# Attention values: three of six key tiles multiplied in one full precision matmul instead of two rounded ones

## The reference

```python
    mask = q_bucket[:, :, :, None] == k_bucket[:, :, None, :]
    scores = scale * np.matmul(q, k.transpose(0, 1, 3, 2))
    scores = np.where(mask, scores, -1000000000.0)
    scores = scores - np.max(scores, axis=-1, keepdims=True)
    attn = np.exp(scores)
    attn = attn / (np.sum(attn, axis=-1, keepdims=True) + 1e-09)
    return np.matmul(attn, v).astype(np.float32)
```

## Time and profile before

| what | value |
|---|---|
| three runs | 1694.59, 1698.58, 1700.28 us |
| their median | 1698.58 us |
| profiled execution, first to last instruction (span) | 1694.0 us |
| lowest of the three runs less that span | 0.6 us |
| mean granted TensorE clock | 0.980 of full |
| attention stage | about 20 to 298 us of the span |

### The profile page before, as it was taken

How to read it: one execution, slowest core, us unless ns; L and a number is a source line. 1 busy time by engine, 2 the same in 40 slices (tenths; PEclk the granted TensorE clock), 3 DMA queues, 4 the chain that set the end, 5 groups by cost and what they waited for, 6 DMA issues and landing times.

```text
span 1694.0 us, 21627 instructions
## 1 busy us (share of the span) xinstructions
PE 1591.6 (94%) x7588; PEld 1310.1 (77%) x7589; DVE 670.9 (40%) x1227; ACT 505.0 (30%) x943; POOL 309.6 (18%) x381
## 2 busy tenths in 40 slices
PE   7999998789999999999999999999999992699997
PEld 6888887568888888888888888888888871577775
DVE  6999998541211211211221121121122134554324
ACT  5887877301111111111111111111111133643213
POOL 3333341320030030030030030030030004322202
PEclk9999999999999999999999999999999995899999
DMA  5343343110110110020020020010011013753310
GB/s 136 92 119 93 104 124 123 51 50 1 50 50 1 50 50 0 15 84 0 0 99 0 0 99 0 0 65 34 0 50 50 1 50 131 271 176 133 134 43 23
DMA packets 49380, 108.06 MB, mean 64 GB/s; under 512 B 7350, under 2 KB 13494, under 8 KB 49344
## 3 DMA queue, kind: packets, MB, share of 16 engines
q1 hardware_dynamic: 44208, 96.30, 17.3%
q10 hardware_dynamic: 2736, 4.98, 1.0%
q0 software_dynamic: 2400, 6.31, 1.0%
HBM read 81.58 MB, written 13.40 MB: 56 GB/s over the span
## 4 chain that ended last, share of the span: by engine, by line
PE 80%; DVE 7%; issue 5%; ACT 3%; DMA 3%; POOL 2%; DVEq 0%; ACTq 0%; POOLq 0%; SPq 0%
PE psum L353 24%; PE psum L355 23%; PE psum L354 23%; PE psum L576 2%; DVE pt_lo L1069 2%; DMA w_raw<-in_moe_w_dram 2%; DVE row_max L1079 1%; PE psum L528 1%; ACT prob L846 1%; PE psum L784 1%; PE psum L565 1%; ACT pt_hi L839 1%; PE psum L566 1%; PE psum L589 1%; PE psum L590 1%
## 5 line engine op out<-in xcount | busy, mean ns | idle before, releaser
L936 ACT ACTIVATE h_hi<-psum 128x512 fp32r<-128x512 f32 x192 | 114.9, 599 | 871.8 <-PE psum L355 871.8
L353 PE MATMUL psum<-xt_lo,w_hi 128*128 128x512 f32 x768 | 304.8, 397 | 0.0
L355 PE MATMUL psum<-xt_hi,w_lo 128*128 128x512 f32 x768 | 301.6, 393 | 0.0
L353 PE MATMUL psum<-w_lo,h_hi 128*128 128x512 f32 x768 | 299.5, 390 | 1.6 <-issue 1.6
L354 PE MATMUL psum<-xt_hi,w_hi 128*128 128x512 f32 x768 | 299.4, 390 | 0.0
L355 PE MATMUL psum<-w_hi,h_lo 128*128 128x512 f32 x768 | 299.1, 390 | 0.0
L354 PE MATMUL psum<-w_hi,h_hi 128*128 128x512 f32 x768 | 298.8, 389 | 0.0
L1232 DVE SCALAR_TENSOR_TENSOR h_lo<-psum,h_hi 128x512 fp32r<-128x512 f32 x192 | 132.7, 691 | 347.9 <-ACT h_hi L936 347.5
L1262 DVE SCALAR_TENSOR_TENSOR tok<-psum,route,tok 128x512 f32<-128x512 f32 x96 | 65.7, 745 | 436.4 <-PE psum L355 436.4
L379 POOL CAST w_hi<-w_raw 128x512 fp32r<-128x512 f32 x64 | 39.2, 612 | 813.4 <-PE psum L355 813.4
L355 PEld LDWEIGHTS psum<-xt_hi,w_lo 128*128 128x128 f32 x768 | 144.6, 188 | 33.8
(11 more groups left out here) (227 smaller groups left out, 2020.5 us busy)
## 6 DMA issues: line engine op xcount, KB each, us to landing
w_raw<-in_moe_w_dram SPq DMA_DIRECT2D x32, 2048.0 KB, 8.0
k_hh<-k_t SPq DMA_DIRECT2D x32, 192.0 KB, 4.0
x_sorted<-zeros SPq DMA_DIRECT2D x21, 257.0 KB, 4.6
x_row<-x_sorted ACTq DMA_DIRECT2D x19, 256.0 KB
k_raw<-in_k_dram SPq DMA_DIRECT2D x16, 192.0 KB, 2.4
q_raw<-in_q_dram SPq DMA_DIRECT2D x16, 192.0 KB, 2.5
v_raw<-in_v_dram SPq DMA_DIRECT2D x16, 192.0 KB, 3.7
k_b<-k_t SPq DMA_DIRECT2D x16, 192.0 KB, 4.3
```

The source lines that it names most:

```text
L353: pe.matmul(acc, a[0], b[1], start=start, stop=False)
L355: return pe.matmul(acc, a[1], b[0], start=False, stop=stop)
L936: act.activation(h_s[0][:, f, :], psum[:, f % 4, :], ACT.Relu).then_inc(m1.h_hi, 1)
```

## The change

The rounded and rest parts `pt_hi` and `pt_lo` are kept only for key tiles 0 to 2. Key tiles 3 to 5 are copied by ScalarE without rounding into a new float32 tile `pt_b`, VectorE's residue for them falls away, and their two rounded matmuls become one plain float32 matmul per key tile. The bank of key tiles 3 to 5 is released by ScalarE's copy instead of VectorE's residue.

```diff
-    pt_hi = [place(f"pt_hi{u}", [P, IT, HALF], F32R, at) for u in range(2)]
-    pt_lo = [place(f"pt_lo{u}", [P, IT, HALF], F32R, at) for u in range(2)]
+    pt_hi = [place(f"pt_hi{u}", [P, IT // 2, HALF], F32R, at) for u in range(2)]
+    pt_b = [place(f"pt_b{u}", [P, IT // 2, HALF], F32, at) for u in range(2)]
+    pt_lo = [place(f"pt_lo{u}", [P, IT // 2, HALF], F32R, at) for u in range(2)]
...
                 if not at_first(g):
-                    pe.wait_ge((s_lo_a, s_lo_b)[c], g)
+                    pe.wait_ge((s_lo_a, s_hi_b)[c], g)
...
             if part == 0:
-                pe.wait_ge(s_lo_b, 3 * hn + 3)
+                pe.wait_ge(s_lo_a, 3 * hn + 3)
+                pe.wait_ge(s_hi_b, 3 * hn + 3)
                 pe.wait_ge(s_v_split, n + 1)
                 pe.wait_ge(s_o_t, hn + 1)
             for j in (2 * part, 2 * part + 1):
+                if j >= IT // 2:
+                    mm = pe.matmul(psum[:, 6, 0:HALF], v_s[u][:, j, :].bitcast(F32), pt_b[half][:, j - IT // 2, :],
+                                   start=False, stop=(j == IT - 1))
+                    continue
                 pe.matmul(psum[:, 6, 0:HALF], v_s[u][:, j, :], pt_lo[half][:, j, :], start=(j == 0), stop=False)
-                mm = pe.matmul(psum[:, 6, 0:HALF], v_s[u][:, j, :], pt_hi[half][:, j, :], start=False,
-                               stop=(j == IT - 1))
+                mm = pe.matmul(psum[:, 6, 0:HALF], v_s[u][:, j, :], pt_hi[half][:, j, :], start=False, stop=False)
...
-                act.copy(pt_hi[half][:, 3 * c:3 * c + 3, a:a + P],
+                act.copy((pt_hi, pt_b)[c][half][:, :, a:a + P],
                          psum[:, 4 + c, 0:HALF].rearrange("p (j i) -> p j i", j=3)).then_inc((s_hi_a, s_hi_b)[c], 1)
...
-            for c in range(2):
-                dve.wait_ge((s_hi_a, s_hi_b)[c], g + 1)
-                dve.tensor_tensor(pt_lo[half][:, 3 * c:3 * c + 3, a:a + P],
-                                  psum[:, 4 + c, 0:HALF].rearrange("p (j i) -> p j i", j=3),
-                                  pt_hi[half][:, 3 * c:3 * c + 3, a:a + P].bitcast(F32),
-                                  ALU.subtract).then_inc((s_lo_a, s_lo_b)[c], 1)
+            dve.wait_ge(s_hi_a, g + 1)
+            dve.tensor_tensor(pt_lo[half][:, :, a:a + P],
+                              psum[:, 4, 0:HALF].rearrange("p (j i) -> p j i", j=3),
+                              pt_hi[half][:, 0:3, a:a + P].bitcast(F32),
+                              ALU.subtract).then_inc(s_lo_a, 1)
```

More of the change, by code:

```diff
@@ L183, in program @@
     s_hi_a, s_hi_b = sem("pt_hi_a"), sem("pt_hi_b")
-    s_lo_a, s_lo_b = sem("pt_lo_a"), sem("pt_lo_b")
+    s_lo_a = sem("pt_lo_a")
     s_pv = sem("values_part")
```

## The result

| | before | changed |
|---|---|---|
| median of the runs | 1697.53 us (4 runs) | 1712.86 us (4 runs) |
| ratio, 95% interval | | 1.0091 [1.0072, 1.0110] |
| span of the profiled execution | 1694.0 us | 1710.1 us |
| mean granted clock | 0.980 | 0.978 |

The change makes the kernel slower by 0.9%, 15.3 us between the medians. The forecast was 1719.4 us, in a range from 1710 to 1732, slower. One of the four changed runs, at 2049.52 us and a granted clock of 0.746, was disturbed: it is not in the ratio, but it is in the median, which is 1712.34 us without it.

A forecast was written before the change was run, and what follows sets the result against it. In attention, VectorE and TensorE were both near their limit, VectorE costing TensorE about one wait per head. Dearer matmuls less waits made +1.30 us per head, +20.8 over 16 heads: span 1714.8, plus 4.6 gives 1719.4 us, range 1710 to 1732.

The forecast's parts named there:

- 12.7 x 2.21: VectorE in the attention stage after the change: 12.7 query-tile steps of 2.21 us, given as about 29 of 40 us.
- step 2: Third of a head's six query-tile steps on TensorE: its 0.59 us wait for pt_lo goes, 2.65 becomes 2.72 us.
- step 3: Fourth query-tile step of a head: copy of o_t no longer hidden in VectorE's delay, 3.10 becomes 3.28 us.
- X: Price on TensorE of one full-precision 384-column value matmul: taken as 0.67 us, 0.32 more than the two rounded ones.
- two clocks per column: Assumed rate of a full matmul's records on TensorE: 384 columns in 320 ns, nearest to the estimated 1.7 and 1.8.
- the 13 ns: Time a rounded matmul has beside its 160 ns of columns, added to 320 ns for a full matmul's record.
- the dear record: Rival: a full matmul costs 0.84 us on TensorE, +16 us over the forecast, 1736 us; chance 0.06.
- 1.30 us per head, 16 heads: Attention stage: a head's six steps grow from 17.65 to 18.95 us on TensorE, together +20.8 us.
- Cheap records: Rival: a full matmul costs 0.345 us, like two rounded ones; -3.5 us, 1695.1 us; chance 0.05.
- All waits were VectorE's: Rival: freeing VectorE dissolves all TensorE waits in the attention stage, 17.5 us per head, 1697 us; chance 0.04.
- VectorE costs TensorE roughly one wait per head: Attention stage: VectorE causes one 0.59 us TensorE wait; the others are ScalarE's copies between dependent matmuls.
- step 5: Last query-tile step of a head on TensorE: two full matmuls, turns begin unwaited, 2.98 becomes 3.52 us.

The follow-up runs named there:

- e12: Kernel before without VectorE's addition of 1e-9 to the row sums, value matmuls not reordered: heads 17.25 us, ratio 1.0000.
- e9: Kernel before with only the value matmuls issued early, ahead of work waiting for ScalarE's copy o_raw: heads 17.48 us, ratio 0.9997.
- e3: Changed kernel with all six key tiles unrounded and multiplied in full precision, no residue on VectorE: 1736.31 us, ratio to before 1.0248.
- e1: Changed kernel, but key tiles 3 to 5 still take two rounded matmuls each, residue gone: heads 17.30 us, ratio to before 0.9989.
- e11: Kernel before with value matmuls issued early and without VectorE's addition of 1e-9 to the row sums: 1686.84 us, ratio 0.9956.

## Why the prediction was right, and where it was off

**Right: the direction and the mechanism.** TensorE pays, VectorE's relief isn't worth it. VectorE was forecast at about 29 of 40 us and is at 29.2 (102.14 of 140), though the prediction's own 12.7 x 2.21 makes 28.1: it took off 0.51 us per step for 0.46, and put the heads too long. The steps forecast for the head of the earlier trace rows and measured in its counterpart: 3.66 and 3.67; 3.07 and 3.05; 2.72 and 2.64; 3.28 and 3.19; 2.70 and 2.67; 3.52 and 3.50. The wait of step 2 is gone, and the one for o_t has come, but it didn't cost what I said: the turn of k still starts 1.98 us after the step (1.99 before), since that is ScalarE's copy in either case. The 0.09 by which step 3 grew lie behind it, between the turn of k and the values: 0.41 us from start to start (233.24 and 233.65), 0.30 before (222.96 and 223.26). The change gave TensorE one more wait there, for `s_lo_a` and `s_hi_b` where before it waited for `s_lo_b` alone. The two kernels with VectorE relieved tell them apart; relief alone, with the added wait:

```profile
220.28 0.54 PE L529 MATMUL psum<-ident,k_s 128*128 128x128 f32 x3
220.69 0.44 PE L596 MATMUL psum<-pt_lo,v_s 128*128 128x384 f32 x1
```

and e12, without it:

```profile
219.95 0.54 PE L528 MATMUL psum<-ident,k_s 128*128 128x128 f32 x3
220.25 0.44 PE L589 MATMUL psum<-pt_lo,v_s 128*128 128x384 f32 x1
```

In the mean of twelve heads it is 0.38 us with the added wait and 0.31 without. So the prediction's step 3 was wrong in its cause as well as in its size: the copy of o_t didn't delay the turn of k, and the semaphores of the values, put down as nothing because both were reached a step earlier, probably cost 0.1 us here by being one more. No run changes that wait alone, so this cause isn't shown.

**The price.** X, the time of one full matmul, was taken as 0.67 us between bounds of 0.345 and 0.84 and measured 0.645. Six full matmuls at 0.025 less are 0.15 us per head, 2.4 us. The choice of two clocks per column held; the 13 ns that I added to each record are 2 or 3. The Trainium skill's rule ("FP8 and Floating Point Precision", TensorE Precision Notes: four passes for a true FP32 matmul) would have given 0.64 as an estimate (4 x 0.16), and the trace agrees with its 0.645, which shows the time and not what the passes are. The cheap and the dear record are both refuted by the same lines.

**The sum.** Forecast +20.8 us for the span, measured +16.1. The mis-sized step is "1.30 us per head, 16 heads". First, the head I walked grew by 18.72 - 17.65 = 1.07 us: of the 0.23 that are missing, 0.15 are the price and 0.09 the wait given to step 3. It is the slower of two that alternate (17.65 and 17.35 before; 18.73 and 18.52 after), and the other grew by 1.17. The mean of two is (240.62 - 203.37)/2 - (211.91 - 176.91)/2 = 18.63 - 17.50 = 1.13 (1.11 by the twelve heads): 2.7 us less over 16.

Second, the stage has ends: from its first to its last turns of probabilities it grew by 289.04 - 274.02 = 15.0 us and not 18.1. The last two heads grew by 0.5 and 0.1 us only; that they prepare no successors, and so have waits which cover some of the price, is my reading and not shown. The first one, which got shorter by 0.3 us, started at half clock in the profile of before and at full clock in the other.

Third, two things that no step of mine holds: the first turns came 1.15 us earlier and the way to the experts took 2.1 us longer. 15.0 - 1.15 + 2.1 = 16.0 of 16.1. These two belong to single executions and not to the change: the first turns start at 20.47 us in before, at 19.15 in e9 and at 20.46 in e3, and the way took 14.6 us in e12 and 16.9 in e3, always with the same work. So about 1 us by which the measured span came nearer to the forecast is luck.

**The rivals.** Cheap records: false by the price. "All waits were VectorE's": false, since relief alone gives 17.30 and not 15.7 (e1). But my own wording, "VectorE costs TensorE roughly one wait per head", was half the truth: right for what this change could gain, wrong as a picture of VectorE, whose loop with TensorE's step 5 was a bound of its own, 0.18 us above the other (e9, and e1 with 17.30). It did no harm to the forecast because the price made TensorE the bound by a margin of 1.1 us per head. It did harm to the next forecast, the reordering of before.

## What to carry to other kernels

Trading VectorE work for TensorE work pays only as long as TensorE has true gaps, and a full float32 matmul of 384 columns costs 0.645 us against 0.345 for two rounded ones: with two engines at their limits, each 0.46 us taken from VectorE was bought for 0.30 us on TensorE and used by nobody. When an engine shows 94% busy with many short instructions, look at the gaps between its starts before you call the rest slack, and follow the one wait that is left to what it waits for: it may close a loop over two engines; and when one relief brings nothing, try it together with a relief of the other bound before you drop it. Look also for an instruction whose length doesn't fit its size: here an addition to three numbers took 824 ns in the median, where one of the residues that the change removed takes 552.

## What the hardware showed that I had not expected

A VectorE instruction on three numbers per partition (SBUF to SBUF, one tensor operand and a constant) lasts 155 ns alone and up to 1032 ns beside a GpSimd tensor_tensor of 384 elements, ending 0.02 us after it (208.11 and 208.09 us). The reciprocal of the same three numbers never exceeded 179 ns, not even in e11, where 19 of its 32 start while GpSimd is at work. Nor did residues or maxima, which read PSUM, show such a stretch (at most 560 and 958 ns in the kernel before). The addition isn't the only victim: row_bias, which takes two tensors of SBUF, lasts 159 ns in the median but up to 468 in the kernel before and 552 in the changed one, each time beside a GpSimd instruction. row_scale, a tensor_scalar as well but on one number, never exceeded 156 ns, though 31 of its 96 in the kernel before start while GpSimd is at work. The Trainium skill ("GPSIMD Engine Reference", Specifications) says that GpSimd shares SBUF interfaces with VectorE and that the two contend where a VectorE instruction runs in a 2-port mode or has two SBUF inputs; that fits row_bias with its two inputs, and the reciprocal with its one. Which form the addition ran in, and why row_scale escapes, no run here shows. How often it is stalled is a matter of timing: in the changed kernel, whose VectorE comes to it at other moments, the addition's median is 160 ns, while row_bias is stretched 23 times of 96, 10 before.
